# A spectral mix and two Strassen feed-forward layers on one core: layer 2's weights split beside layer 1, and more values held in PSUM

## What is computed

```python
Yr = Xr @ w_r - Xi @ w_i + b_r;  Yi = Xr @ w_i + Xi @ w_r + b_i
Yr, Yi = soft_threshold(Yr, 0.01), soft_threshold(Yi, 0.01)
x = irfft(Yr + 1j * Yi)
# layer 1: 256 -> 2048 -> 256
h = x @ w_in;  g = max(h, 0) + alpha * min(h, 0);  x = g @ w_out
# layer 2: 256 -> 2048 -> 256
h = x @ w_in2; g = h if h >= 1, 0 if h <= -1, else (h + 1) ** 2 / 4;  out = g @ w_out2
```

## Time and profile before

| | us |
|---|---|
| median of 3 runs | 1236.69 |
| lowest, highest | 1234.26, 1238.33 |
| the profiled execution: its time | 1238.44 |
| its span, first to last instruction | 1236.6 |
| PE, DVE, ACT, POOL busy in the span | 1183.2, 1000.4, 855.8, 726.4 |

### The profile page before, as it was taken

The page is one execution under the profiler, slowest core; times in us unless marked ns, Lnnn a source line. Parts: engine busy times, 40 slices in busy tenths (PEclk is TensorE's granted clock), DMA queues, the critical chain, the costliest instruction groups (busy, mean ns, idle before and its releaser), DMA issues. The chain is left out here.

```text
span 1236.6 us, 21167 instructions
## 1 busy us (share of the span) xinstructions
PE 1183.2 (96%) x6944; PEld 1139.8 (92%) x6944; DVE 1000.4 (81%) x1711; ACT 855.8 (69%) x1874; POOL 726.4 (59%) x676
## 2 busy tenths in 40 slices
PE   7899989999999999999998898999999999999996
PEld 2788879999999999999997887899999999999996
DVE  2578788888888888787889998788888888888874
ACT  2334547777777777676766687787878787878774
POOL 0005545656565656566668787675757575757553
PEclk9899999999999999999999999999999999999999
DMA  9677630101000001000001110100000000000001
GB/s 283 186 243 227 201 94 2 26 1 26 2 26 2 26 1 26 1 27 1 18 1 35 35 35 18 23 5 19 8 19 8 17 10 19 9 17 10 17 10 26
DMA packets 54534, 54.41 MB, mean 44 GB/s; under 512 B 30132, under 2 KB 42548, under 8 KB 54420
## 3 DMA queue, kind: packets, MB, share of 16 engines
q1 hardware_dynamic: 51786, 46.57, 13.5%
q10 hardware_dynamic: 2638, 6.49, 1.5%
HBM read 34.29 MB, written 18.74 MB: 43 GB/s over the span
## 5 line engine op out<-in xcount | busy, mean ns | idle before, releaser
L459 POOL TENSOR_TENSOR g_lo<-g_sb,g_hi 128x376 fp32r<-128x376 f32 x512 | 555.7, 1088 | 374.9 <-ACT g_hi L686 370.0
L1060 PE MATMUL bank<-g_hi,w_out_hi 128*128 128x376 f32 x1024 | 343.3, 335 | 10.4 <-POOL g_lo L459 10.1
L1060 PE MATMUL bank<-g_hi,w_out_lo 128*128 128x376 f32 x1024 | 342.7, 335 | 0.0
L1060 PE MATMUL bank<-g_lo,w_out_hi 128*128 128x376 f32 x1024 | 341.6, 334 | 0.0
L1060 PE MATMUL bank<-xc_hi,w_in_hi 128*128 128x376 f32 x896 | 304.7, 340 | 11.1 <-DVE partial L838 9.0
L1060 PE MATMUL bank<-xc_hi,w_in_lo 128*128 128x376 f32 x896 | 300.8, 336 | 0.0
L1060 PE MATMUL bank<-xc_lo,w_in_hi 128*128 128x376 f32 x896 | 299.1, 334 | 0.0
L686 ACT ACTIVATE g_hi<-g_sb 128x376 fp32r<-128x376 f32 x512 | 259.8, 507 | 15.5 <-DVE g_sb L876 8.1
L876 DVE SCALAR_TENSOR_TENSOR g_sb<-act_a,neg_alpha,g_sb 128x376 f32<-128x376 f32 x256 | 230.7, 901 | 0.9 <-ACT g_sb L673 0.8
L1060 PEld LDWEIGHTS bank<-g_hi,w_out_hi 128*128 128x128 f32 x1024 | 192.4, 188 | 15.8 <-POOL g_lo L459 9.7
L1060 PEld LDWEIGHTS bank<-g_lo,w_out_hi 128*128 128x128 f32 x1024 | 193.2, 189 | 0.0
(11 more groups left out here) (75 smaller groups left out, 1411.8 us busy)
## 6 DMA issues: line engine op xcount, KB each, us to landing
slots_scratch<-a_sb ACTq DMA_DIRECT2D x16, 384.0 KB, 4.7
gc<-group_consts SPq DMA_DIRECT2D x24, 256.0 KB, 3.7
zt<-slots_scratch SPq DMA_DIRECT2D x24, 256.0 KB, 4.3
inverse_scratch<-v_sb SPq DMA_DIRECT2D x24, 256.0 KB, 3.6
ut<-inverse_scratch SPq DMA_DIRECT2D x16, 384.0 KB, 4.5
x_sb<-x SPq DMA_DIRECT2D x16, 320.0 KB
out<-yt SPq DMA_DIRECT2D x124, 32.0 KB, 1.6
raw_in_sb<-wpack SPq DMA_DIRECT2D x8, 256.0 KB, 3.7
```

The lines of the kernel that those rows point to most:

```text
L459: pool.tensor_tensor(g_lo[kind][:, :], g_sb[n % 3][:, :], g_hi[kind][:, :].bitcast(f32), ALU.subtract)\
L1060: done = pe.matmul(out_ap, w, g, start=first and n == 0, stop=last_one and n == 2, skip_group_check=unchecked)
```

## The change

1. Layer 2's weights are split during layer 1, in 16 jobs m (chunk n = m // 2; even m: w_in, odd: w_out), one every three groups from group 4. POOL makes an even job's sums in group 4 + 3m; in group 5 + 3m ACT writes the hi part to `prep_hi`, POOL the lo part in place in two halves, and SP stores both to DRAM scratch. The hi and lo slices are loaded from there in groups 56 to 64, each when its old content has been used for the last time. `take_sums`, `take_in_hi`, `take_out_hi`, `take_in_lo`, `take_out_lo` and SP's raw loads are gone.
2. Blocks C21 and C12 of h are written in place into their banks, only C22 goes to SBUF (`h22`). p7 and p5 of the next group wait for the second part of that block instead of its sum. In layer 1, Relu(-h) is written in place over h (a bank for three of the four blocks), behind Relu(h); act_a isn't used there.
3. Order: on PE p5 stands behind the out product of C21 (was before it). On DVE C22 stands behind second part C11 and the tokens. On ACT high C11 stands before first C22. In group 0 inverse(47) stands before p7.
4. y_clip is kept in bank 3. gc has four slots, so that pair p waits for pair p - 4. SP loads a pair's two token tiles in the first group of the pair before, both after all its token jobs.

```diff
@@ -50,9 +50,10 @@
-TAKE_IN = {1: 0, 2: 1, 3: 2, 5: 3, 7: 4, 9: 5, 11: 6, 13: 7}
-TAKE_OUT = {3: 0, 5: 1, 7: 2, 9: 3, 11: 4, 13: 5, 14: 6, 15: 7}
+PREP_FROM, PREP_EVERY = 4, 3
 TAKE_FROM = LAYER_GROUPS - FP
+GC_SLOTS = 4
@@ -270,11 +277,13 @@
-        def taken(table, g):
-            return table.get(g - TAKE_FROM)
+        def prep_job(g, part):
+            m, at = divmod(g - PREP_FROM - part, PREP_EVERY)
+            return (m, m // 2, m % 2) if at == 0 and 0 <= m < 2 * FP else (None, None, None)
         def h_of(kind):
-            return c11_bank[:, 0:N] if kind == C11 else h_sb[kind][:, :]
+            return h22[:, :] if kind == C22 else {C11: c11_bank, C21: c21_bank, C12: c12_bank}[kind][:, 0:N]
@@ -299,9 +308,10 @@
             def load_matrices(p):
-                if p >= SLOTS:
-                    sp.wait_ge(inv_done, 2 * p - 4)
-                sp.dma_start(gc[p % SLOTS][:, :], group_consts[p % (GROUPS // 2), :, :]).then_inc(gc_in[p % SLOTS], 16)
+                if p >= GC_SLOTS:
+                    sp.wait_ge(inv_done, 2 * (p - GC_SLOTS) + 2)
+                sp.dma_start(gc[p % GC_SLOTS][:, :], group_consts[p % (GROUPS // 2), :, :])\
+                  .then_inc(gc_in[p % GC_SLOTS], 16)
@@ -371,26 +381,54 @@
-            for t in range(2, TILES):
-                sp.wait_ge(side_done, 4 * (t // 2 - 1) + (4 if t % 2 == 0 else 3))
+            def load_tokens(t):
+                sp.wait_ge(side_done, 4 * (t // 2))
                 if t == TILES_PER_BATCH:
...
-            for g in range(2 * FP):
...
+            def load_prep(m):
+                if m:
+                    sp.wait_ge(prep_stored, 32 * m)
+                else:
+                    sp.wait_ge(wout_lo_ready, FP)
+                n, cols = m // 2, slice(0, 4 * P) if m % 2 == 0 else slice(4 * P, 4 * P + 2 * D)
+                sp.dma_start(prep_raw[:, 0:512], wpack[1, n, :, cols]).then_inc(prep_in, 16)
+            def store_prep(m):
+                n = m // 2
+                sp.wait_ge(prep_hi_ready, m + 1)
+                sp.wait_ge(prep_lo_ready, 2 * m + 2)
+                if m % 2 == 0:
+                    sp.dma_start(win_z[n, 0, :, :], prep_hi[:, :].bitcast(f32)).then_inc(prep_stored, 16)
+                    sp.dma_start(win_z[n, 1, :, :], prep_raw[:, P:]).then_inc(prep_stored, 16)
+                else:
+                    sp.dma_start(wout_z[n, 0, :, :], prep_hi[:, 0:2 * D].bitcast(f32)).then_inc(prep_stored, 16)
+                    sp.dma_start(wout_z[n, 1, :, :], prep_raw[:, 0:2 * D]).then_inc(prep_stored, 16)
+            load_prep(0)
+            for g in range(TAKE_FROM):
+                q, at = divmod(g, FP)
+                if at == 0:
+                    load_tokens(2 * q + 2)
+                    load_tokens(2 * q + 3)
+                m = prep_job(g, 1)[0]
+                if m is not None:
+                    store_prep(m)
+                    if m + 1 < 2 * FP:
+                        load_prep(m + 1)
+            sp.wait_ge(prep_stored, 32 * 2 * FP)
+            for n in range(FP + 1):
+                if n < FP:
+                    sp.wait_ge(p3_done, TAKE_FROM + n + 1)
+                    sp.dma_start(w_in_hi[:, n, :].bitcast(f32), win_z[n, 0, :, :]).then_inc(win_in[n], 16)
+                    sp.dma_start(w_in_lo[:, n, :].bitcast(f32), win_z[n, 1, :, :]).then_inc(win_in[n], 16)
+                if n:
+                    sp.wait_ge(out_done, out_no(TAKE_FROM + n - 1, C12) + 1)
+                    sp.dma_start(w_out_hi[:, n - 1, :].bitcast(f32), wout_z[n - 1, 0, :, :]).then_inc(wout_in[n - 1], 16)
+                    sp.dma_start(w_out_lo[:, n - 1, :].bitcast(f32), wout_z[n - 1, 1, :, :]).then_inc(wout_in[n - 1], 16)
@@ -459,22 +497,31 @@
-            def take_in_lo(g, part):
...
+            def prep_sums(g):
+                m, n, is_out = prep_job(g, 0)
+                if m is None or is_out:
+                    return
+                pool.wait_ge(prep_in, 16 * (m + 1))
+                blocks = prep_raw[:, :].rearrange("p (k c) -> p k c", k=W + 1)
+                a21, a11, a12 = blocks[:, 0, :], blocks[:, 1 + A11, :], blocks[:, 1 + A12, :]
+                a22 = blocks[:, 1 + A22, :]
+                pool.tensor_tensor(blocks[:, 1 + S1, :], a21, a22, ALU.add).then_inc(s1_made, 1)
+                pool.tensor_tensor(blocks[:, 1 + S3, :], a11, a21, ALU.subtract)
...
+            def prep_low(g, part):
+                m, n, is_out = prep_job(g, 1)
+                if m is None:
+                    return
+                size = D if is_out else W * P // 2
+                cols = slice(part * size, (part + 1) * size)
+                whole = prep_raw[:, 0:2 * D] if is_out else prep_raw[:, P:]
+                pool.wait_ge(prep_hi_ready, m + 1)
+                pool.tensor_tensor(whole[:, cols].bitcast(f32r), whole[:, cols], prep_hi[:, cols].bitcast(f32),
+                                   ALU.subtract).then_inc(prep_lo_ready, 1)
@@ -505,11 +552,11 @@
                 lows_first(q + 1, at)
-                take_in_lo(g, 0)
+                prep_low(g, 0)
                 low(g - 1, C12)
                 lows_second(q + 1, at)
-                take_in_lo(g, 1)
-                take_out_lo(g)
+                prep_low(g, 1)
+                prep_sums(g)
                 if g < ALL_GROUPS:
@@ -663,16 +710,16 @@
                     act.wait_ge(h_ready[kind], g + 1)
-                if n >= 2:
-                    act.wait_ge(g_ready, n - 1)
-                a, gg = act_a[n % 2][:, :], g_sb[n % 3][:, :]
+                h, gg = h_of(kind), g_sb[n % 3][:, :]
                 if g < LAYER_GROUPS:
-                    act.activation(a, h_of(kind), ACT.Relu, scale=-1.0)
                     if n >= 3:
                         act.wait_ge(lo_ready, n - 2)
-                    act.activation(gg, h_of(kind), ACT.Relu).then_inc(act_done, 1)
+                    act.activation(gg, h, ACT.Relu)
+                    act.activation(h, h, ACT.Relu, scale=-1.0).then_inc(act_done, 1)
                 else:
-                    act.activation(a, h_of(kind), ACT.Relu, bias=half[:, 0:1], scale=0.5).then_inc(root_ready, 1)
+                    act.wait_ge(g_ready, n - 1)
+                    a = act_a[n % 2][:, :]
+                    act.activation(a, h, ACT.Relu, bias=half[:, 0:1], scale=0.5).then_inc(root_ready, 1)
                     act.wait_ge(root_ready, n - 4 * LAYER_GROUPS + 1)
@@ -695,18 +742,18 @@
-            def take_in_hi(g):
-                n = taken(TAKE_IN, g - 1)
-                if n is not None:
+            def prep_high(g):
+                m, n, is_out = prep_job(g, 1)
+                if m is None:
+                    return
+                if m:
+                    act.wait_ge(prep_stored, 32 * m)
+                if is_out:
+                    act.wait_ge(prep_in, 16 * (m + 1))
+                    act.activation(prep_hi[:, 0:2 * D], prep_raw[:, 0:2 * D], ACT.Copy).then_inc(prep_hi_ready, 1)
+                else:
                     act.wait_ge(s_made, FP + n + 1)
-                    act.activation(w_in_hi[:, n, :], raw2_in[n % 2][:, P:], ACT.Copy).then_inc(win_hi_ready, 1)
...
+                    act.activation(prep_hi[:, :], prep_raw[:, P:], ACT.Copy).then_inc(prep_hi_ready, 1)
@@ -725,8 +771,8 @@
                 if g < ALL_GROUPS:
+                    high(g, C11)
                     first_part(g, C22)
-                    high(g, C11)
                 if at == 0:
@@ -775,12 +821,12 @@
                 dve.wait_ge(y_sum_ready, s + 1)
-                dve.tensor_scalar(y_clip[:, :], y_sum[:, :], LAM, -LAM, ALU.min, ALU.max)\
+                dve.tensor_scalar(clip_bank[:, 0:D], y_sum[:, :], LAM, -LAM, ALU.min, ALU.max)\
                    .then_inc(y_clip_ready, 1)
...
                     dve.wait_ge(inv_done, s - 2)
-                dve.tensor_tensor(y_out[s % SLOTS][:, :], y_sum[:, :], y_clip[:, :], ALU.subtract).then_inc(y_ready, 1)
+                dve.tensor_tensor(y_out[s % SLOTS][:, :], y_sum[:, :], clip_bank[:, 0:D], ALU.subtract).then_inc(y_ready, 1)
@@ -847,23 +893,22 @@
-            def make_h(g, kind, begun, bank_of):
-                if g:
-                    dve.wait_ge(g_ready, block_no(g - 1, kind) + 1)
-                dve.tensor_tensor(h_sb[kind][:, :], begun[:, :], bank_of[:, 0:N], ALU.add).then_inc(h_ready[kind], 1)
-
             def make_c22(g):
...
                 dve.wait_ge(u3_ready, g + 1)
-                make_h(g, C22, partial, c12_bank)
+                if g:
+                    dve.wait_ge(g_ready, block_no(g - 1, C22) + 1)
+                dve.tensor_tensor(h22[:, :], partial[:, :], c12_bank[:, 0:N], ALU.add).then_inc(h_ready[C22], 1)
...
                 dve.wait_ge(p4_done, g + 1)
-                make_h(g, C21, u2, c21_bank)
+                h = h_of(C21)
+                dve.tensor_tensor(h, u2[:, :], h, ALU.add).then_inc(h_ready[C21], 1)
...
                 dve.wait_ge(p3_done, g + 1)
-                make_h(g, C12, u2, c12_bank)
```

(66 more changed lines are left out.)

51 lines of the change are left out of this document (9 added, 42 removed).

## The result

The changed kernel takes **1214.83 us** in the median of 4 runs (1214.68 to 1215.00), the kernel before 1235.9; the ratio is 0.9828, 95% interval 0.981 to 0.9846. Forecast were 1213 and 1201 to 1228. The profiled execution took 1215.0 with a span of 1213.2.

What follows compares the result with a forecast made beforehand. PE's own pace bounds both layers except at the border; the transform also has waits. From 1236.69 us: border -27.9, jobs +8, PE's order +2.4, group 0 +0.7, transform -7, giving 1213; range 1201 to 1228.

Steps and rivals of the forecast that it cites:

- The border: Groups 56 to 71: without taking layer 2's weights there, 124.7 us instead of 152.6, a gain of 27.9 us.
- The jobs: Splitting layer 2's weights beside layer 1 makes some g_lo late on POOL: +8 us, from 0 to 20.
- the sums: POOL's sums in token groups 4 and 28 (0.45 us late each), 22 and 46 (1.15 each): 3.2 us.
- the halves: POOL's two w_in_lo halves in token groups 5, 11, 29, 35 make g_lo of C11 late: 4 x 1.25 = 5 us.
- The transform: Transform stage: y_clip and y_out steady at 0.42 us with operands in PSUM, curing PE's waits: -7 us, -3 to -11.
- PE's order: Later p5 on PE: slack 0.3 us, nothing lost in ordinary groups; +2.4 us at layer 2's pair borders, -3 to +6.
- rival 2: Late p5's loop through g_lo of C21 outlasts PE's group; layer 2's eights above 63 us; total 1251 us; chance 6%.
- Both Relus behind the wait three blocks back: Layer 1, ACT: both Relus of a block wait for an earlier g_lo, making the next g_hi some 0.4 us later.
- Operands in PSUM: DVE's second parts with h in banks: three of four steady at 0.54 to 0.60 us, hidden behind PE, worth 0.
- 1 (every part of a job late, 1231): Layer 1: jobs push g_lo by 1.1 us in all 24 parts, +26 instead of +8, 1231 us; chance 12%.
- 3 (jobs free and 10 in the transform, 1202): POOL's lows absorb all jobs (0 for 8) and the transform gains 10: 1202 us; chance 22%.
- 4 (weights late): Border: DRAM weights arrive late or a stall of its own remains, half the gain lost, 1227 us; chance 6%.

Runs made afterwards that it cites:

- b1: The kernel before without taking layer 2's weights (their loads and waits left out; layer 2 computes with layer 1's weights): 1209.3 us, ratio 0.9768.
- a1: The changed kernel without the 16 jobs and 32 weight loads (layer 2 computes with layer 1's weights): 1209.9 us, ratio 0.9776 to the kernel before.
- a5: The changed kernel with y_clip back in an SBUF tile: 1221.0 us, ratio 0.9865 to the kernel before.
- a6: The changed kernel with three slots of matrices (gc) instead of four: 1216.1 us, ratio 0.9825 to the kernel before.
- a2: The changed kernel with p5 back in front of the out product of C21: 1202.9 us, ratio 0.9719 to the kernel before.
- a8: The changed kernel with C21 and C12 of h in SBUF and p5 back before the out product of C21: 1213.2 us, ratio 0.9806.
- a7: The changed kernel with C21 and C12 of h in SBUF tiles, p5 still late: 1236.3 us, ratio 0.9987 to the kernel before.
- a4: The changed kernel with p5 before the out product of C21 and POOL's second half and sums behind g_lo of C11: 1200.5 us, ratio 0.9699.

## Why the prediction was right, and where not

**The border: right.** The forecast -27.9 came as -28.0, and b1 shows that its cause was the weights' work alone. The loads come in time: 0, as put. The new order lost 1.0 of it again (a1 against b1); 62.34 us for eight groups, from which the sum was made, already held the old order's loss at the borders of pairs, and so the total came out.

**The jobs: right in mechanism; right in size for the sums, too high for the halves.** Forecast 8, measured 6.6 (a1). A late g_lo of C11 is waited for in the next group. From p1 to p1 and against a1, groups 5 and 29, behind the sums in 4 and 28, are longer by 0.5 each, and groups 23 and 47, behind those in 22 and 46, by 1.0 to 1.1: together 3.1 us, where 3.2 were put. Behind the two halves, groups 6 and 30 are longer by 0.9 to 1.0 and 12 and 36 by 0.5: 2.9 us, where 5 were put. Groups 17, 18 and 42 have 0.6 in all, which the sum had at nothing. The chain that ended last runs through both kinds, first the four sums in front of g_lo of C11 of group 4, then the order that was worked out for group 5, activation, half, g_lo of C12, token, half, g_lo of C11:

```profile
208.50 0.42 POOL prep_raw L508
208.92 0.42 POOL prep_raw L509
209.34 0.74 POOL prep_raw L511
...
210.15 0.46 POOL prep_raw L513
210.61 0.96 POOL g_lo L497
...
211.62 1.29 PE bank L1089 x6
...
214.19 0.95 ACT prep_hi L756
...
215.21 1.16 POOL prep_raw L523
...
216.39 1.01 POOL g_lo L497
217.39 0.96 POOL xc_lo L472
218.35 1.11 POOL prep_raw L523
219.47 1.27 POOL g_lo L497
```

Group 5 begins with p1 at 210.14, and PE's two waits are

```profile
210.14 0.33 PE L1089 MATMUL bank<-xc_hi,w_in_hi 128*128 128x376 f32 x1
...
211.61 0.19 PEld L1089 LDWEIGHTS bank<-g_hi,w_out_hi 128*128 128x128 f32 x1 [0.60 <-POOL g_lo L497]
...
220.78 0.19 PEld L1089 LDWEIGHTS bank<-g_hi,w_out_hi 128*128 128x128 f32 x1 [0.59 <-POOL g_lo L497]
```

The last g_lo ends at 220.74, 10.6 us into the group, where 10.5 was worked out. PE wanted it later than was put, since group 5 was itself longer by the wait before. Group 0 is longer by 1.1, where inverse(47) was put at 0.7; a1, without jobs, has that too.

**The transform: right in cause and about in size.** -6.3 for -7; over the other profiles with y_clip in a bank it lies between -2.9 and -6.7. y_clip and y_out were its cause (a5), the matrices' slots were not (a6). Of the 5.6 + 3.9 us of waits that were to be cured, y_out's fell to 0.8, but xt_lo's stayed at 3.5. A part was given back: PE's wait for zt, 0.8 us in the kernel before, is 2.1 here. That the steps ahead of it are quicker and the load is not would explain it; no run shows it. From 110 to 140 us PE waited on DMA once (total, times, longest):

```profile
PE bank L1043 <- DMA zt<-slots_scratch: 2.1, 1, 2.1
```

**PE's order: wrong, and this is the step that failed.** It said: slack 0.3 in layer 2, so 0 in an ordinary group, and 2.4 us more behind the borders of pairs. Measured is the reverse. From p1 to p1, a border of pairs costs PE 0.6 us (8.3 for 7.7, in the second group of a pair), as much as before (8.0 for 7.7 in two groups). But every second ordinary group takes 7.9 us instead of 7.7, all through layer 2 except in its last pair. The loop in the changed kernel goes from the end of one g_lo of C21 over out product C21, p5, the sum of C22, its activation and the g_hi to the end of the next g_lo of C21. These are two turns of it, in groups 100 and 101:

```profile
980.43 1.01 POOL L497 TENSOR_TENSOR g_lo<-g_sb,g_hi 128x376 fp32r<-128x376 f32 x1 [0.47 <-ACT g_hi L733]
...
983.38 0.55 DVE L901 TENSOR_TENSOR h<-partial,bank 128x376 f32<-128x376 f32 x1 [0.35 <-PE bank L1089]
...
985.15 1.10 DVE L925 SCALAR_TENSOR_TENSOR g_sb<-h,act_a 128x376 f32<-128x376 f32 x1 [0.70 <-ACT act_a L724]
...
986.29 0.52 ACT L733 ACTIVATE g_hi<-g_sb 128x376 fp32r<-128x376 f32 x1 [0.15 <-DVE g_sb L925]
...
988.37 1.01 POOL L497 TENSOR_TENSOR g_lo<-g_sb,g_hi 128x376 fp32r<-128x376 f32 x1 [0.47 <-ACT g_hi L733]
...
991.27 0.55 DVE L901 TENSOR_TENSOR h<-partial,bank 128x376 f32<-128x376 f32 x1 [0.52 <-PE bank L1089]
...
994.03 0.52 ACT L733 ACTIVATE g_hi<-g_sb 128x376 fp32r<-128x376 f32 x1
...
996.10 1.00 POOL L497 TENSOR_TENSOR g_lo<-g_sb,g_hi 128x376 fp32r<-128x376 f32 x1 [0.47 <-ACT g_hi L733]
```

| part of the loop | put at | group 100 | group 101 |
|---|---|---|---|
| g_lo of C21 there, to DVE's sum of C22 (PE: out C21, p5) | 4.85 + 7.72 - 10.8 = 1.77 | 983.38 - 981.44 = 1.94 | 991.27 - 989.38 = 1.89 |
| sum of C22 to g_hi of C22 | 7.53 - 4.85 = 2.68 | 986.29 - 983.38 = 2.91 | 994.03 - 991.27 = 2.76 |
| g_hi of C22 to the end of g_lo of C21 | 10.5 - 7.53 = 2.97 | 989.38 - 986.29 = 3.09 | 997.10 - 994.03 = 3.07 |
| loop | 7.42 | 7.94 | 7.72 |

The first part had been put too low, 1.77 for 1.9. And `second_part` of C22 on DVE, the only one that still has both operands in SBUF, takes 0.9 to 1.1 us in five of a pair's eight groups instead of 0.55, so that g_hi of C22 waits for it and the middle part of the loop grows by up to 0.26. In groups 122 to 125 of the last pair, where nothing is made for a next pair, that operation takes 0.55. There the later two parts of the loop are 2.66 and 3.00, as they were put; with a first part of 1.9 the loop would be 7.56, and the groups take 7.76. So the bare loop has 0.2 us of slack, not 0.3, and the one stretched operation takes more than that in every second group. That is rival 2's loop, at its threshold rather than 0.7 beyond; eight groups took 62.9 us, just under the 63 that were named as its sign. In a2 p5 no longer waits for that product. There the first part can be as short as 1.3, that operation of C22 stays under 0.6 us, and 7.8 us come back in groups 72 to 127. In layer 1 the late p5 costs 2.9 beside the jobs (a2); what it costs there without them no run shows, since a1 and b1 differ in banks and group 0 as well. Both Relus behind the wait three blocks back, which was put into the jobs' sum, and the new places of C22 on DVE and of high C11 on ACT were not run by themselves either.

Behind a pair's border the chain that ended last goes through the same loop, with the late g_lo at its end:

```profile
763.59 0.62 ACT act_a L722
...
768.39 1.01 POOL g_lo L497
...
769.44 56.49 PE bank L1089 x324
```

**Operands in PSUM: mis-sized.** Put at 0 in the steady groups; measured are 4.8 + 3.8 us beside the early p5 (a2 against a8) and about 21 beside the late one (a7 against the changed kernel). The prediction had the late p5 and the plain durations together and never worked out that the first needs the second. The second part of layer 2 takes 530 ns at least from a bank and 549 from SBUF. The Trainium skill's 58 and 120 cycles ("VectorE: DVE Perf Modes", "The TRN2 errata") would have made the bank the slower one by an estimated 65 ns; these rows don't show it.

**The rivals.** 1 (every part of a job late, 1231): no, the eights with jobs take 65.3 to 67.3 us, not over 68. 3 (jobs free and 10 in the transform, 1202): no; a4 reaches 1200.5, with the jobs nearly free, but the rest of its gain is PE's order in layer 2 and not the transform. 4 (weights late): no, a1 has the same border without loads.

The sum came out near for the reasons stated at the border, in the jobs and in the transform. Part is luck: 4.0 us too little for PE's order in ordinary groups was made up for by 2.4 too much at the borders and 2.1 too much for the jobs' halves.
